# Copies of the transposed v on ScalarE instead of VectorE, and a new order of the first batch's steps around v and phi

## What is computed

```python
# attention over pooled keys: q, k, v are (8, 8, 576, 64)
k_p = k.reshape(B, H, 72, 8, D).mean(axis=3); v_p = v.reshape(B, H, 72, 8, D).mean(axis=3)
attn = softmax(q @ k_p.T / sqrt(D));  x = attn @ v_p          # x: (4608, 512)
# soft mixture of experts, 8 experts x 4 slots
logits = x @ phi                                              # phi: (512, 32)
d = softmax(logits, axis=0); slot_input = d.T @ x
slot_out[e] = relu(slot_input[e] @ w1[e]) @ w2[e]
x = softmax(logits, axis=1) @ slot_out
# h = x @ w_in; solu = h * softmax(h); out = layer_norm(solu) * g_ln @ w_out
```

## Time and profile before

| | us |
|---|---|
| median of 3 runs (lowest, highest) | 463.44 (461.39, 463.53) |
| the profiled execution | 462.13 |
| its span, first to last instruction | 460.3 |
| busy: TensorE, VectorE, ScalarE, GpSimd | 439.4, 322.3, 262.5, 256.5 |
| first batch begins, repeated batches, last batch's work ends | 8.5, 46 to 166, 187 |

### The profile page before, as it was taken

One profiled execution on the slowest core, in us unless ns is written; L12 is line 12 of the kernel. 1 busy time (PEld: TensorE's weight loads), 2 busy tenths in 40 slices (PEclk: granted clock), 3 DMA queues, 4 the chain that ended last, 5 costly groups with the idle time before them and its releaser, 6 DMA issues.

```text
span 460.3 us, 10081 instructions
## 1 busy us (share of the span) xinstructions
PE 439.4 (95%) x3537; PEld 340.8 (74%) x3537; DVE 322.3 (70%) x543; ACT 262.5 (57%) x583; POOL 256.5 (56%) x348
## 2 busy tenths in 40 slices
PE   6678999999999998999999999999999999999996
PEld 5566778788787885545568888788888888888874
DVE  5788786878778694745579987677777777777311
ACT  2567668787776854315368754555555555566210
POOL 3758887867878421102014426666666666666540
PEclk9999999999999999999999999999999999999999
DMA  8969999798979567999800065666666666666652
GB/s 251 296 178 257 378 265 289 290 250 314 313 248 279 191 255 273 344 376 398 325 1 23 29 133 93 136 132 135 135 135 135 136 137 136 135 134 137 129 124 46
DMA packets 125582, 91.71 MB, mean 199 GB/s; under 512 B 104936, under 2 KB 104944, under 8 KB 123632
## 3 DMA queue, kind: packets, MB, share of 16 engines
q1 hardware_dynamic: 125552, 91.32, 71.9%
HBM read 66.13 MB, written 9.44 MB: 164 GB/s over the span
## 4 chain that ended last, share of the span: by engine, by line
PE 39%; SPq 38%; DVE 7%; DMA 6%; issue 5%; ACT 3%; POOL 1%; DVEq 0%; ACTq 0%
SPq L483 32%; PE banks L1228 7%; DMA wslot<-in_moe_w 4%; PE banks L1285 4%; SPq L472 3%; PE banks L1216 3%; PE banks L1301 3%; PE banks L1337 3%; PE banks L1473 2%; PE banks L1309 2%; PE banks L1604 2%; PE banks L1606 2%; PE banks L1605 2%; PE banks L1495 2%; DMA ql<-in_q 1%
## 5 line engine op out<-in xcount | busy, mean ns | idle before, releaser
L1604 PE MATMUL banks<-wo_hi,uh 128*128 128x512 f32 x288 | 112.8, 392 | 0.4 <-POOL ul L601 0.4
L1605 PE MATMUL banks<-wo_lo,uh 128*128 128x512 f32 x288 | 112.1, 389 | 0.0
L1606 PE MATMUL banks<-wo_hi,ul 128*128 128x512 f32 x288 | 112.1, 389 | 0.0
L601 POOL TENSOR_TENSOR ul<-u_col,uh 128x1024 fp32r<-128x1024 f32 x30 | 72.1, 2405 | 31.6 <-ACT uh L628 31.6
L524 POOL TENSOR_TENSOR attn<-attn,srec 128x576 f32<-128x576 f32 (+1 forms) x40 | 45.9, 1147 | 40.9 <-DVE srec L927 40.8
L844 ACT ACTIVATE sq<-u,usum 128x1024 f32<-128x1024 f32 x36 | 41.5, 1154 | 41.5 <-DVE u L1144 41.5
L1604 PEld LDWEIGHTS banks<-wo_hi,uh 128*128 128x128 f32 x288 | 54.1, 188 | 12.5 <-issue 1.0
L1606 PEld LDWEIGHTS banks<-wo_hi,ul 128*128 128x128 f32 x288 | 54.1, 188 | 11.4
L1605 PEld LDWEIGHTS banks<-wo_lo,uh 128*128 128x128 f32 x288 | 54.1, 188 | 11.0
L1134 DVE TENSOR_REDUCE nmax<-banks 128x1 f32<-128x1024 f32 x36 | 43.5, 1218 | 17.5 <-PE banks L1581 16.0
L1144 DVE SCALAR_TENSOR_TENSOR u<-banks,ex 128x1024 f32<-128x1024 f32 x36 | 43.8, 1222 | 14.9 <-ACT ex L837 14.8
(11 more groups left out here) (178 smaller groups left out, 737.4 us busy)
## 6 DMA issues: line engine op xcount, KB each, us to landing
wslot<-in_moe_w SPq DMA_DIRECT2D x13, 2048.0 KB, 10.0
u_col<-u_blk SPq DMA_DIRECT2D x240, 64.0 KB, 2.1
qb<-in_q SPq DMA_DIRECT2D x32, 256.0 KB, 6.2
out<-osb SPq DMA_DIRECT2D x32, 256.0 KB, 2.6
vraw<-in_v SPq DMA_DIRECT2D x8, 640.0 KB, 5.4
kraw<-in_k SPq DMA_DIRECT2D x7, 640.0 KB, 9.5
vraw<-in_v SPq DMA_DIRECT2D x8, 512.0 KB, 4.2
kraw<-in_k SPq DMA_DIRECT2D x7, 512.0 KB, 7.8
```

The lines of the kernel that those rows point to most:

```text
L601: pool.tensor_tensor(ul[par][:, :, :].rearrange("p c (q t) -> p (c q) t", q=4), v, uh[par][:, :, :].bitcast(F32).rearrange("p c (q t) -> p ...
L1604: pe.matmul(ps[4 + par], uh[par][:, c, :], wo_hi[:, c, :], start=(c == 0), stop=False)
L1605: pe.matmul(ps[4 + par], uh[par][:, c, :], wo_lo[:, c, :], start=False, stop=False)
L1606: last = pe.matmul(ps[4 + par], ul[par][:, c, :], wo_hi[:, c, :], start=False, stop=(c == FC - 1))
```

## The change

`vT_close` moves from VectorE to ScalarE. On VectorE it stood in step 4 for the next batch (and in step 1 for batch 0); on ScalarE it stands at the end of step 1 of each batch for that same batch, behind the copies of aT. In batch 0 it stands behind the copy of qT in step 1. For batch 0 alone three orders change: TensorE multiplies v by phi for batch 0 ahead of the scores of tile 3; for batch 1 it does so in step 5 behind scores, instead of at the end of step 4; and ScalarE's `vT_evac` for batch 1 stands behind the copy of lt in step 4 and not ahead of it.

```diff
 # ScalarE
+            def vT_close(b):
+                act.wait_ge(sem("vT_sb"), b + 1)
+                for hh in range(2):
+                    c = 1 + hh * HEAD
+                    last = copy(vT[hh * D:(hh + 1) * D, :, :], vpad[hh * D:(hh + 1) * D, :, c:c + SP])
+                last.then_inc(sem("vT_closed"), 1)
...
-                if t == 4 and not last:
+                if t == 4 and not last and not first:
                     vT_evac(b + 1)
                 if first:
-                    if t != 1:
+                    if t == 1:
+                        vT_close(b)
+                    else:
                         lt_evac(ahead(b, par, t - 1))
+                    if t == 4:
+                        vT_evac(b + 1)
                     aT_evac(tile, 0)
...
                 aT_evac(tile, 1)
+                if t == 1:
+                    vT_close(b)
 # VectorE
-            def vT_close(b):
-                dve.wait_ge(sem("vT_sb"), b + 1)
...
-                if t == 1 and first:
-                    vT_close(b)
-                if t == 4 and not last:
-                    vT_close(b + 1)
 # TensorE
+                if t == 1 and first:
+                    wphi_t(b)
                 if not (last and t + 2 >= TILES):
                     scores(ahead(b, par, t + 2))
+                if t == 5 and first:
+                    wphi_t(b + 1)
...
                 if t == 1 and first:
-                    wphi_t(b)
                     vphi_t(b)
                     aT_t(tile)
...
-                if t == 4 and not last:
+                if t == 4 and not last and not first:
                     wphi_t(b + 1)
```

## The result

The changed kernel took 464.05 us (median of 19 runs, 462.7 to 467.35), the kernel before 462.64 (19 runs beside them, 461.3 to 465.11). The ratio is 1.0034, 95% interval 1.0021 to 1.0047: slower by 1.6 us, inside the half per cent that was called no change. The forecast was 0.3 us slower. The profiled executions differ by 1.3 us of span (461.6 against 460.3), and what follows divides that difference. A few executions fell into a slower state (one of 495 us of the kernel with the repeated pairs on VectorE, 463.5 and 464.1 us of the one with all three repairs); the ratios leave these out, the medians do not.

What follows compares the result with a forecast made beforehand. TensorE was taken to bound the repeated batches and late VectorE the first. A front gain of 4.0 us against 4.35 lost in five batches gave +0.3 on the 463.44 median: 463.8 us, range 460.6 to 466.3.

Steps and rivals of the forecast that it cites:

- The bound: TensorE binds the repeated batches, so waits before it cost full length; in the first batch VectorE is late.
- The steady term: Batches 1 to 6: the pair on ScalarE costs 0.87 us in each of batches 2 to 6, 4.35 us together.
- The slack: Repeated batches, ScalarE from lt of tile 0 to lt of tile 1: nil, so the pair's delay goes through whole.
- The front term: First batch, vT pairs gone from VectorE and orders changed: batch 1's v72 4.0 us earlier, range 3.0 to 5.0.
- the second rival: First batch: another wait takes VectorE's place, front gives only 1.5 us, 466.3 us in all; chance 0.16.
- Phi ahead: First batch, product with phi ahead of tile 3's scores: VectorE's vphi copies start at 23.1, a gain of 0.7 us.
- The 0.9 wait for the lt copy of tile 4: First batch: TensorE, done with aT at 38.1, waits 0.9 us for ScalarE's copy before vphi's transposes.
- Batch 7: Last batch: no kblk copies, ScalarE idle 1.02 us before lt, which covers the pair's 0.87; no cost.
- The sum: Whole kernel: batch 1 4.0 us earlier, batches 2 to 6 4.35 later, together +0.3 us, 463.8 us.
- a front gain of 2.1: First batch: the gain under which the kernel would be slower by more than 0.5% (2.3 us).
- The first: Repeated batches: the pair on ScalarE costs nothing, 458.5 us, half a stall 461.1; chance of none or half 0.17.
- The third: GpSimd holds the copies on ScalarE too; 1 us more in each of six batches gives 470 us; chance 0.05.

Runs made afterwards that it cites:

- all three repairs: The change with the pair ahead of lt of tile 0, normalisation behind VectorE's add, and batch 0's steps 4 and 5 in old order: 458.13 us, ratio 0.9910.
- the pair in a gap: The change, but in batches 1 to 7 ScalarE makes its vT pair ahead of lt of tile 0: 459.01 us, ratio 0.9925.
- the first of the two with the change's pairs: The change, but batch 0's product with phi behind the scores of tile 3, first profiled of two: 464.71 us, ratio 1.0050.
- the pairs alone: The kernel before, with only the vT pairs of batches 0 and 1 on ScalarE and all orders old: 460.67 us, ratio 0.9955.
- the repeated batches' part alone: The kernel before, with the vT pair of batches 1 to 7 on ScalarE behind aT of tile 1: 466.14 us, ratio 1.0076.
- the added wait for the add: The change, with GpSimd's normalisation of tile 3 waiting for VectorE's second-level add of v for batch 1: 464.03 us, ratio 1.0040.

## Why the prediction was right

*The bound.* In the repeated batches "a wait put before TensorE costs its full length": shown three ways. The pair behind aT costs 0.89 a batch, twice the pair 1.8 in the batches with a full clock, the pair in a gap 0.09.

*The steady term.* 4.35 forecast, 4.43 measured. The pair was taken at 0.87 for no overlap; its 16 copies have a median of 0.439 (0.434 forecast from the line of two other forms), and 0.89 for two. The Trainium skill, "ScalarE: Activation LUTs", section "What ACT_TABLE_LOAD costs", has neighbours overlap: the estimate of 0.76 worked out from its figures would have given 3.8. The trace differs, the second copy starts where the first ends, and the measurement decides. The slack was nil, as forecast, and nothing was made up: v72 keeps its 0.58 behind the lt copy, and the lag grows batch by batch.

*The front term.* 4.0 forecast, 3.05 measured, at the lower end of its range. The step that was mis-sized: "the ones after them some 3.2 earlier; VectorE's two v folds start when GpSimd's add ends". They did, at 28.90, but the first was priced at the 0.81 of a quiet moment. Moved earlier it met GpSimd's normalisation, which had started 0.08 before, and took 1.75. That is the second rival on a small scale, though not by the waits it named: another wait did take the place of the one removed, worth 0.8 of the 1.0 us at batch 1's v72. The rest, about 0.2, is not traced. "SBUF — State Buffer" of the Trainium skill has the rule, in the section "Who interferes with whom": a VectorE instruction with two SBUF inputs also contends with a GpSimd instruction that reads SBUF. The traces agree (1.75 beside the normalisation, 0.82 without).

*The orders.* Phi ahead: 0.7 forecast until VectorE's vphi copies, which did start at 23.13; 0.3 to 0.6 of it reaches batch 1, as far as single executions tell. The 0.9 wait for the lt copy of tile 4 was there (0.76). That the new order of steps 4 and 5 costs about 0.2 against the old one was not part of the forecast.

*Batch 7.* Nothing, as forecast: the pair lies in the 1.02 of idle time, of which 0.24 is left.

*The sum.* The forecast was the small difference of two large terms, 4.35 less 4.0; the measured one is 4.43 less 3.05, 1.4 us at the end of attention instead of 0.3. The sign held. That the time stayed inside the half per cent with a front 1.0 us short is room in the forecast, which counted on it down to a front gain of 2.1, and not precision.

*The rest.* The shift did not pass quite one to one: v72 of batch 7 is 1.38 late, the last expert product 1.62 (226.48 against 224.86), the end of the span 1.3. Such tenths lie within what executions differ by, as tile 3's scores above show.

*Rivals.* The first (no cost in the repeated batches) fell by the distances. The second (a front gain of 1.5) did not come to pass at 3.05. The third (copies held on ScalarE too) fell: 16 copies between 0.432 and 0.442, GpSimd at work or not.

## What to carry to other kernels

An engine that is idle a quarter of the time can still be the one that everything waits for in one stretch: look for the row of its instructions without a gap that ends in the full engine's wait, and put a new piece ahead of the instruction that the row starts with, where the engine still waits, and not into the row. Here the same two copies cost 4.4 us in one place and 0.45 a few us earlier in the batch. And when a stall goes, the pieces behind it move beside other neighbours: price them again there, above all those of VectorE beside GpSimd's.

## What the runs showed of the hardware that was not expected

The granted clock fell to 1.2 GHz in the middle of busy work, with stalls well under 2 us. With the pair twice it fell behind idle times of 1.58 and 1.59 us, in three of six batches, at 1.6 to 1.7 us of loss each; a like stall in the other batches (1.58 to 1.61) had no such effect, nor had the 0.67 of the change in any batch.

In the first batch it was at 0.50 from 26 to 30 in three profiles, all of kernels with phi's product behind the scores (the first of the two with the change's pairs, the pairs alone, the repeated batches' part alone). TensorE had idled there ahead of vphi's transposes, as in this row of the pairs alone, and twice for 0.2 to 0.4 behind it:

```profile
22.52 0.55 PE L1275 MATMUL banks<-ident,wphi 128*128 128x128 f32 x3 [1.29 <-ACT wphi L628]
```

A repeat of the first and the kernel before have the same waits and kept 1.00 in their profiles. All eight kernels with phi ahead and batch 0's pair on ScalarE kept 1.00 in the whole first batch; the one with phi ahead and the pair on VectorE had 0.50 from 32 to 35, behind 1.43 of idle time, which the kernel before had too and kept 1.00. So the new place of phi's product may be worth more than its 0.3 to 0.6 us, by keeping the clock up. The mean clocks of the timed executions do not settle it: under 0.997 are 29 of 66 of the kernel before and 3 of 10 with phi's product behind the scores, but 2 of 19 of the change, 3 of 10 with the added wait for the add, and 5 of 9 with phi ahead and the old order in steps 4 and 5. They do not say where the clock fell, and this stays open.
